# Second layer in groups of 512 tokens, rows turned straight from the stored first-layer result

## The reference, cut to what matters

```
h = x @ w_in1 ;  x2  = (h - tanh(h)) @ w_out1
h = x2 @ w_in2 ; sp = log1p(exp(min(h, 20)))
out = (h * tanh(sp)) @ w_out2
```

## Time and profile before

| what | us |
|---|---|
| median of 3 runs (lowest, highest) | 484.51 (483.85, 485.36) |
| the profiled execution's own time | 483.82 |
| its span, first to last instruction | 482.0 |
| TensorE busy, share of the span | 450.0, 93% |
| VectorE busy | 357.0, 74% |
| ScalarE busy | 240.8, 50% |
| GpSimd busy | 157.0, 33% |

### The profile page before, as it was taken

How to read it: one execution, slowest core, us unless ns; L and a number is a source line. 1 busy time by engine, 2 the same in 40 slices (tenths; PEclk the granted TensorE clock), 3 DMA queues, 4 the chain that set the end, 5 groups by cost and what they waited for, 6 DMA issues and landing times.

```text
span 482.0 us, 9558 instructions
## 1 busy us (share of the span) xinstructions
PE 450.0 (93%) x3517; PEld 435.7 (90%) x3517; DVE 357.0 (74%) x638; ACT 240.8 (50%) x400; POOL 157.0 (33%) x115
## 2 busy tenths in 40 slices
PE   7859799999999999999998999995999999999996
PEld 7759789999999999999998998895999998989995
DVE  8886969578596777856547568779768877797774
ACT  4436324522632442452265467665676567656770
POOL 1363432332132142232212304235423542354334
PEclk9767969999999999999999999998999999999999
DMA  6994134017014202900005330000000000000000
GB/s 159 295 247 145 46 90 92 2 46 182 0 44 135 46 1 88 256 12 0 2 2 136 105 110 0 1 1 28 2 1 27 0 27 0 0 27 0 27 1 27
DMA packets 26730, 29.07 MB, mean 60 GB/s; under 512 B 13952, under 2 KB 19856, under 8 KB 26704
## 3 DMA queue, kind: packets, MB, share of 16 engines
q1 hardware_dynamic: 26704, 28.72, 21.4%
HBM read 26.71 MB, written 2.01 MB: 60 GB/s over the span
## 4 chain that ended last, share of the span: by engine, by line
PE 42%; issue 32%; POOL 15%; SPq 4%; DVE 3%; DMA 3%; POOLq 0%; ACT 0%; ACTq 0%
PE bank L995 16%; PE bank L987 16%; POOL act_lo L415 14%; PE bank L955 3%; DMA qs<-q_t 3%; PE bank L930 3%; PE bank L942 2%; POOL act_lo L229 1%; SPq L270 1%; DVE wi_lo L286 1%; PE bank L965 1%; SPq L318 1%; PE bank L971 1%; SPq L307 0%; DVE og L657 0%
## 5 line engine op out<-in xcount | busy, mean ns | idle before, releaser
L987 PE MATMUL bank<-x_lo,wi_hi 128*128 128x256 f32 x576 | 156.9, 286 | 0.0
L995 PE MATMUL bank<-wo_hi,act_hi 128*128 128x320 f32 x384 | 124.3, 324 | 6.1 <-POOL act_lo L415 3.3
L995 PE MATMUL bank<-wo_lo,act_hi 128*128 128x320 f32 x384 | 119.7, 312 | 0.0
L995 PE MATMUL bank<-wo_hi,act_lo 128*128 128x320 f32 x384 | 119.6, 312 | 0.0
L415 POOL TENSOR_TENSOR act_lo<-hid,act_hi 128x512 fp32r<-128x512 f32 x48 | 76.2, 1586 | 126.8 <-DVE act_hi L859 126.8
L987 PE MATMUL bank<-x_hi,wi_hi 128*128 128x256 f32 x384 | 114.6, 299 | 0.2 <-DVE hid L847 0.2
L987 PEld LDWEIGHTS bank<-x_lo,wi_hi 128*128 128x128 f32 x576 | 112.3, 195 | 0.0
L229 POOL TENSOR_TENSOR act_lo<-act,act_hi 128x512 fp32r<-128x512 f32 x42 | 55.3, 1316 | 174.2 <-ACT act_hi L463 166.9
L987 PE MATMUL bank<-x_hi,wi_lo 128*128 128x256 f32 x384 | 110.0, 286 | 0.0
L995 PEld LDWEIGHTS bank<-wo_hi,act_hi 128*128 128x128 f32 x384 | 73.3, 191 | 9.6 <-issue 6.4
L987 PEld LDWEIGHTS bank<-x_hi,wi_hi 128*128 128x128 f32 x384 | 74.9, 195 | 2.8 <-issue 0.9
(11 more groups left out here) (93 smaller groups left out, 612.0 us busy)
## 6 DMA issues: line engine op xcount, KB each, us to landing
stage<-w_out SPq DMA_DIRECT2D x8, 640.0 KB, 5.8
decay<-neg_top_rows SPq DMA_DIRECT2D x10, 512.0 KB, 4.2
stage<-w_in SPq DMA_DIRECT2D x8, 512.0 KB, 4.3
stage<-w_in SPq DMA_DIRECT2D x16, 128.0 KB, 5.6
ks<-k_t SPq DMA_DIRECT2D x12, 160.0 KB
qs<-q_t SPq DMA_DIRECT2D x12, 160.0 KB
kt<-k_tok SPq DMA_DIRECT2D x6, 320.0 KB, 4.2
v<-v_tok SPq DMA_DIRECT2D x6, 320.0 KB, 5.3
```

The lines of the kernel that those rows point to most:

```text
L987: last = pe.matmul(dst, w, x, start=(n == 0), stop=(n == len(parts) - 1))
L995: last = pe.matmul(acc[b][:, 0:DM], a[:, t], w[:, j, :], start=(first and n == 0), stop=(last_tile and n == 2))
```

## The change

The second layer works in G2 = 3 groups of NT = 4 tiles of 128 tokens (512 tokens). A hidden bank now holds one block of 128 hidden features by 512 tokens; `project_in` has matmuls of 512 columns. The output adds up in four banks (0 to 3), three banks (4 to 6) are left for `hidden2`, bank 7 for the transposes. The 48 blocks t = 16 g + f are cut into 14 batches of the sizes `SIZES`. Rounding to `act2_hi` moves from VectorE to ScalarE, behind the batch's Tanh. `keep` writes the doubled 64 features itself, and the transposes read `x2`, so `gather` is gone. Tiles 0 to 3 are turned in the last group of the first layer, tiles 4 to 11 one per batch at the batches j = 0 to 3 and 5 to 8 (`turning`). ScalarE and VectorE share the copies of the four output tiles; each tile is stored by its own DMA.

```diff
+    G2 = G // 2
+    NT = 2 * NB
+    SIZES = [(2, 4, 4, 4, 2), (4, 4, 4, 4), (4, 4, 4, 2, 2)]
-    hidden2 = bank[4:8]
-    turn2 = bank[2:4]
+    acc2 = bank[0:4]
+    hidden2 = bank[4:7]
+    turn2 = bank[7]
+    def turned_to(i):
+        return bank[4 + i] if i < NT else turn2
+    batches, opens, turning = [], [], {}
+    for g in range(G2):
+        for i, size in enumerate(SIZES[g]):
+            start = batches[-1][-1] + 1 if batches else 0
+            batches.append(range(start, start + size))
+            opens.append(i == 0)
+            if g + 1 < G2 and i < NT:
+                turning[len(batches) - 1] = NT * (g + 1) + i
+    def hidden_of(t):
+        return hidden2[t % 3]
...
 GpSimd
+        for t in range(G2 * FT):
+            pool.wait_ge(high2, t + 1)
+            pool.tensor_tensor(act2_lo[...t...], hid[:, t % PU, :], act2_hi[...t...], ALU.subtract).then_inc(low2, 1)
...
 ScalarE
         def keep(g):
             act_.wait_ge(outs, RING + NP * (g + 1))
             for b in range(NB):
-                last = act_.activation(x2[...], acc[b][:, 0:DM], ACT.Copy)
+                act_.activation(tile[:, 0:DM], acc[b][:, 0:DM], ACT.Copy)
+                last = act_.activation(tile[:, DM:DM + REM], acc[b][:, 2 * P:DM], ACT.Copy)
+        def x2_high_of(i):
+            act_.wait_ge(x2_turned, i + 1)
+            (the two copies of x_high, from turned_to(i))
+        def exps(tiles):
+            for t in tiles:
+                act_.wait_ge(in2_done, t + 1)
+                if t >= PU:
+                    act_.wait_ge(prod2, t + 1 - PU)
+                act_.activation(soft[:, t % PU, :], hidden_of(t)[:, :], ACT.Exp).then_inc(exps2, 1)
+        def highs_of(tiles):
+            for t in tiles:
+                act_.wait_ge(prod2, t + 1)
+                if t >= 2 * PU:
+                    wait_out2(act_, t - 2 * PU)
+                act_.activation(act2_hi[...t...], hid[:, t % PU, :], ACT.Copy).then_inc(high2, 1)
+        for j, tiles in enumerate(batches):
+            exps(tiles)
+            if j in turning:
+                x2_high_of(turning[j])
+            logs_and_tanhs(tiles)
+            if j < 2:
+                split_high(act_, 14 + j)
+            if j and opens[j]:
+                finish(tiles[0] // FT - 1)
+            highs_of(tiles)
+        finish(G2 - 1)
...
 VectorE
+        for j, tiles in enumerate(batches):
+            clips(tiles)                     # t >= PU: waits low2 of t - PU
+            if j in turning:
+                x2_low_of(turning[j])
+            products(tiles)
+            if j < 2:
+                split_low(dve, 14 + j)
+            if j and opens[j]:
+                finish(tiles[0] // FT - 1)
+        finish(G2 - 1)
...
 TensorE
+        def turn_x2(i):
+            if i < NT:
+                pe.wait_ge(kept, NT // NB + 1)
+                pe.wait_ge(sums_read, 2 * G)
+            else:
+                pe.wait_ge(x2_ready, i)
+            for t in range(3):
+                last = pe.transpose(turned_to(i)[:, t * P:(t + 1) * P], x2[:, i, t * P:(t + 1) * P], ident[:, :])
+            last.then_inc(x2_turned, 1)
+        def in_batch(tiles):
+            for t in tiles:
+                f, g = t % FT, t // FT
+                if f == 0:
+                    pe.wait_ge(x2_ready, NT * (g + 1))
+                if t >= 3:
+                    pe.wait_ge(copied2, t - 2)
+                project_in(hidden_of(t)[:, :], f, wi2_hi, wi2_lo, x2_hi[g % 2], x2_lo[g % 2]).then_inc(in2_done, 1)
+        pe.wait_ge(kept, 1 + G)
+        in_batch(batches[0])
+        for j, tiles in enumerate(batches):
+            if j in turning:
+                turn_x2(turning[j])
+            if tiles is not batches[-1]:
+                in_batch(batches[j + 1])
+            else:
+                keep_warm(WARM[3], turn2)
+            out_batch(tiles)                 # per tile: wait low2, then 4 b x 3 matmuls of 320 columns
```

More of the change, by code:

```diff
@@ L357, in _ @@
             load_weights(sp, n)
[L359 to L366, removed]
+        for i in range(2 * G):
+            g, b = i // NB, i % NB
+            sp.wait_ge(final_odd if i % 2 else final_even, i // 2 + 1)
+            sp.dma_start(out[g * L + b * CH * L:g * L + b * CH * L + L, :], out_sb[:, i % NT, :]).then_inc(stored, 16)
+        sp.wait_ge(stored, 16 * 2 * G)
     @block.gpsimd
@@ L409, in _ @@
         steps(G - 1, None)
[L412 to L420, removed]
+        for t in range(G2 * FT):
+            pool.wait_ge(high2, t + 1)
+            pool.tensor_tensor(act2_lo[:, t // PU % 2, t % PU, :], hid[:, t % PU, :], act2_hi[:, t // PU % 2, t % PU, :],
+                               ALU.subtract).then_inc(low2, 1)
     @block.scalar
@@ L483, in steps @@
                     weights_of(c, NQ - 1)
-                if k == NP - 1:
-                    next_high(c, 0)
+                if c is not None and k == NP - 1:
+                    x_high(y_turned, score, 0, 2 * c + 1, y_high)
                 if c is None and k < 4:
@@ L497, in steps @@
                     weights_of(n, 0)
-                if k == NP - 1:
-                    next_high(c, 1)
+                if c is not None and k == NP - 1:
+                    x_high(y_turned, score, 1, 2 * c + 2, y_high)
+                if c is None and 3 <= k < 3 + NT:
+                    x2_high_of(k - 3)
             if n is not None:
@@ L526, in _ @@
         steps(G - 1, None, None)
[L529 to L573, removed]
@@ new lines, in highs_of, with finish @@
+        def highs_of(tiles):
+            for t in tiles:
+                act_.wait_ge(prod2, t + 1)
+                if t >= 2 * PU:
+                    wait_out2(act_, t - 2 * PU)
+                act_.activation(act2_hi[:, t // PU % 2, t % PU, :], hid[:, t % PU, :], ACT.Copy).then_inc(high2, 1)
+        def finish(g):
+            for b in range(0, NT, 2):
+                act_.wait_ge(acc2_done, NT * g + b + 1)
+                if g:
+                    act_.wait_ge(stored, 16 * NT * g)
+                act_.activation(out_sb[:, b, :], acc2[b][:, 0:DM], ACT.Copy).then_inc(final_even, 1)
@@ L721, in residue, with x2_low_of @@
                               ALU.subtract).then_inc(residues, 1)
[L723 to L734, removed]
+        def x2_low_of(i):
+            buf, c = i // NT % 2, slice(i % NT * L, (i % NT + 1) * L)
+            dve.wait_ge(x2_high, i + 1)
+            dve.tensor_tensor(x2_lo[buf][:, :, c], turned_to(i)[:, 0:3 * P].rearrange("p (t n) -> p t n", t=3),
+                              x2_hi[buf][:, :, c], ALU.subtract).then_inc(x2_ready, 1)
         dve.sem_inc(residues, H_BANKS)
@@ L837, in _, with clips, products, finish @@
         steps(G - 1, None, None)
[L840 to L867, removed]
+        def clips(tiles):
+            for t in tiles:
+                dve.wait_ge(in2_done, t + 1)
+                dve.wait_ge(exps2, t + 1)
+                if t >= PU:
+                    dve.wait_ge(low2, t + 1 - PU)
+                dve.tensor_copy(hid[:, t % PU, :], hidden_of(t)[:, :]).then_inc(copied2, 1)
+                dve.tensor_scalar(soft[:, t % PU, :], soft[:, t % PU, :], EXP20, None, ALU.min).then_inc(clipped2, 1)
+        def products(tiles):
+            for t in tiles:
+                dve.wait_ge(tanh2, t + 1)
+                dve.wait_ge(copied2, t + 1)
+                dve.tensor_tensor(hid[:, t % PU, :], hid[:, t % PU, :], soft[:, t % PU, :],
+                                  ALU.mult).then_inc(prod2, 1)
+        def finish(g):
+            for b in range(1, NT, 2):
+                dve.wait_ge(acc2_done, NT * g + b + 1)
+                if g:
+                    dve.wait_ge(stored, 16 * NT * g)
+                dve.tensor_copy(out_sb[:, b, :], acc2[b][:, 0:DM]).then_inc(final_odd, 1)
         split_low(dve, 12)
@@ L1069, in steps, with keep_warm @@
                         attend(c, n, k, 2 + half)
-                if c is None and k == 6:
-                    turn_x2(0, score)
-        def keep_warm(count):
+                if c is None and 2 <= k < 2 + NT:
+                    turn_x2(k - 2)
+        def keep_warm(count, dst=hidden[0]):
             for _ in range(count):
-                pe.matmul(hidden[0][:, 0:P], ones[:, :], ones[:, :], start=True, stop=True)
+                pe.matmul(dst[:, 0:P], ones[:, :], ones[:, :], start=True, stop=True)
         def spread_rows(q):
@@ L1117, in _ @@
         steps(G - 1, None, None)
-        def out_unit(j, half, g, first=False):
-            if half == 0 and not first:
-                pe.wait_ge(final_ready, 2 * g)
-            for p in range(PU):
-                wait_split(pe, 12 + (half * PU + p) // 2, p % 2)
-                pe.wait_ge(low2, PU * j + p + 1)
-                for t in (2 * (half * PU + p), 2 * (half * PU + p) + 1):
-                    last = project_out(act2_hi[:, half, p, :], act2_lo[:, half, p, :], t, wo2_hi, wo2_lo, t == 0,
-                                       t == FT - 1)
```

(44 more changed lines are left out.)

70 lines of the change are left out of this document (44 added, 26 removed).

## The result

The changed kernel takes 529.95 us (median of 4 runs, 528.81 to 531.35) against 484.18 us before (4 runs): ratio 1.0947, 95% interval 1.0917 to 1.0977. The forecast was 534 us, range 512 to 548, slower. The span of its profiled execution is 528.0 us.

A forecast was written before the change was run, and what follows sets the result against it. TensorE's pace was taken as the bound: plain schedule 464.1, plus 49.3 for stand-stills and 18.8 for the clock, gives a 532.2 us span; 1.8 around it and 0.7 more make 534.7, stated as 534, range 512 to 548.

The forecast's parts named there:

- The turned tiles: Second layer: turn behind out(j-1) makes ScalarE wait with batch j half done; TensorE stands still eight times, 49.3 us together.
- The clock: Behind each of eight stand-stills TensorE works 5.1 us at the lower clock, losing 2.35 us each, 18.8 in all.
- Start and end: Second layer: first inward tile at 281.7 us; 4.3 us open at the end; 3.4 us from last matmul to end.
- Matmuls of 512 columns: Inward product: 384 instead of 768 matmuls, 0.227 us each, 13 ns saved per matmul dropped, 5.1 us less.
- The plain schedule of 464.1: Whole kernel if nothing waits for late turns: a span of 464.1 us, 18 us gained.
- The rounding, which I costed at nothing: Rounding moved from VectorE to ScalarE, 2.2 us per full batch, taken as covered by TensorE's work, so zero cost.
- clock stays up: Rival, 20%: TensorE's clock does not fall behind the stand-stills; 516 us.
- only the low part: Rival, 4%: TensorE waits only for the low part, 3 us at some seven places, no lower clock; about 490 us.
- covered: Rival, 5%: ScalarE's late start is covered and only the plain schedule counts; 467 us.

The follow-up runs named there:

- Experiment 1: Changed kernel with only TensorE's order altered: each turn right behind in(j), ahead of out(j-1); 483.78 us, ratio 0.9998 to the kernel before.
- experiment 2: Changed kernel, TensorE's order kept; ScalarE makes x's high parts behind its roundings, VectorE the low part behind its products; 486.16 us, ratio 1.0059 to the kernel before.
- experiment 4: Changed kernel with small filler matmuls (24, 19 or 25 `keep_warm`) in TensorE's eight stand-stills; 516.22 us, 13.7 us below the changed kernel.
- one pair of kernels: Inward matmuls of 512 columns against two of 256: Experiment 1's kernel 0.9998 against 1.0018; the other pair, the joined one, 474.15 against 477.53 us.
- experiment 6: Experiment 1's kernel with batch sizes (4,4,4,4), (4,4,4,4), (4,4,4,2,2), no two-tile batch in front; 475.34 us, ratio 0.9819 to the kernel before.
- experiment 8: Experiment 1's kernel with each inward matmul of 512 columns made as two of 256; 484.7 us, ratio 1.0018 to the kernel before.
- experiment 5: Experiment 1's kernel with the rounding given back to VectorE, behind each product; 506.1 us, ratio 1.0441 to the kernel before.
- the joined one: experiment 6's kernel, last `keep` awaited behind the first inward batch, weight units 14, 15 split ahead of batches 1 and 2's last Exp; 473.79 us, again 474.15.

## Why the prediction was right, point by point

- **The turned tiles**, the step that decides: right in place and mechanism. Experiments 1 and 2 take the wait of ScalarE away from its two sides and end the loss, the second but for 2 us. That ScalarE's waits would be about 6.5 us was too even (five near 7.3, two of 3.2), but TensorE's stand-still counts from the turn and is as long at j = 1 and 5 as elsewhere. The stand-stills in the trace are 4.86, 6.84, 5.70, 6.26, 6.24, 5.61, 5.61 and 3.99 + 1.32 us, 46.4 together against 49.3 forecast. The rows count from the modelled end of a matmul (0.39 long where the next starts after 0.227), so some 0.16 us of each of the eight are missing: 47.7.
- **The clock**: right, the size somewhat over. In windows of 0.5 us the eight stretches of work at the lower level sum to 34 us, 4.2 each and not 5.1 (the one stretch that the forecast went by; from its rows it is 5.2), which makes 15 us of loss by the spacing of the earlier trace rows where I had 18.8; experiment 4 gave back 13.7. The length differs from one stand-still to the next, from 2.8 to 6.0 us, and one stretch was too thin a ground for it. One stretch of 3.2 us at the very end was not foreseen, 1.4 us.
- **Start and end**: first inward tile at 279.9, forecast 281.7. That point lies between 279.9 and 282.2 us in the traces of the eight kernels that have the same work and order ahead of it, so it is no finding. At the end TensorE has 4.5 us between the outward tiles, forecast 4.3: small warm-up matmuls, then a wait for the low part.

```profile
515.44 1.50 PE L1088 MATMUL bank<-ones 128*128 128x128 f32 x12
519.91 0.63 PE L1143 MATMUL bank<-wo_hi,act_hi 128*128 128x320 f32 x1 [2.97 <-POOL act_lo L452]
```

From the last matmul to the end it takes 2.9 us, forecast 3.4. Together: 532.2 - 1.8 - 1.6 + 0.2 - 0.5 - 3.5 + 1.4 = 526.4 against a span of 528.0; 1.6 us I do not place.
- **Matmuls of 512 columns**: the spacing is 0.227 us as worked out. The gain of 5.1 us was right as TensorE's own time; of it 0.9 us showed in one pair of kernels and 3.4 in the other, and what the clock did behind single waits differs by some 1.5 us within each pair.
- **The plain schedule of 464.1** is the step that failed, though it took no part in the result. It assumed that without the late turn nothing would wait. Experiment 1 ended 13 us above the 471 expected. 6.3 us of these are the two stand-stills beside small outward parts (j = 1 and 5) and 4.5 the slower clock behind them and at the end, (3.4 + 3.2 + 3.4) x 0.45; 2.3 more are in the trace only because its first inward tile starts at 282.17 and not at 279.9. In the changed kernel the two lie inside the longer ones at the same places. The rounding, which I costed at nothing "as long as the batch's chain starts when its inward part ends", is part of it: the chain does start there, is not covered, and has 2.2 us of rounding in it.
- The rival "clock stays up" is excluded by the windows, "only the low part" by the releaser of seven of eight waits, and "covered" by the result.

## What to carry to other kernels

When two engines follow orders written by hand, check for each wait what its releaser has queued ahead: here seven groups of three transposes behind the wrong matmuls cost 46 us, and the tiling looked like the culprit. A chain beside TensorE is covered by what TensorE does meanwhile, so a smaller batch at an end also shortens the cover of its neighbour; taking two such batches out was worth 8 us (experiment 6). A long stand-still costs twice, once by itself and once by the clock behind it, here about 47 and 15 us.

## What the runs showed of the hardware that was not expected

- A float32 matmul of 128 columns on `ones` shows as two of 0.114 us each (764 for 382 issued, in 86.8 us), while an fp32r matmul shows as one.
- In the second layer, all of TensorE's waits of 3.2 us and more lowered its clock, in every trace here. Those up to 1.72 us did not. In between it came out both ways: waits of 2.91 us (experiments 1 and 2) lowered it and one of 2.61 (experiment 8) did not, yet one of 2.31 in experiment 5 did, 1.5 us after work had begun again:

```profile
448.33 0.50 PE L996 MATMUL bank<-x_hi,wi_hi 128*128 128x512 f32 x1 [2.31 <-DVE hid L869]
...
450.00:451.00 1.00, 1.00 (x5) 0.50 0.00 0
```

- The same last wait of 2.97 us lowered the clock in the changed kernel and not in the joined one (both its traces) or in experiment 2. With 3.4 us of work at the lower level behind it, that is an estimated 1.5 us by which two executions can differ.
